# A fused decay-attention and two-MLP kernel: the seventh unit's gate moved behind the first MLP block, with the decays, loads and warming products around it reordered

## The reference

```python
f = 1.0 / (1.0 + np.exp(-f_logit))
for t in range(S):
    state = f[:, :, t, :, None] * state + np.einsum('bhd,bhe->bhde', k[:, :, t], v[:, :, t])
    y[:, :, t] = np.einsum('bhd,bhde->bhe', q[:, :, t], state)
...
x = y.transpose(0, 2, 1, 3).reshape(3072, 384)
x = (sigmoid(x @ w_gate) * (x @ w_val)) @ w_out          # d_ff 1536
h = x @ w_in                                             # d_ff 2048
out = (h * sigmoid(1.702 * h)) @ w_out2
```

## Time and profile before

| | |
|---|---|
| median of 3 runs | 955.58 us (955.3 to 957.54) |
| profiled execution, time | 953.83 us |
| its span (first to last instruction) | 952.1 us |
| mean granted TensorE clock | 0.988 of full |
| busy: TensorE, its weight loads | 930.8 us (98%), 778.2 us (82%) |
| busy: VectorE, ScalarE, GpSimd | 457.1 us (48%), 375.9 us (39%), 110.5 us (12%) |
| DMA | 52.36 MB, mean 55 GB/s |

### The profile page before, as it was taken

How to read it: one execution, slowest core, us unless ns; L and a number is a source line. 1 busy time by engine, 2 the same in 40 slices (tenths; PEclk the granted TensorE clock), 3 DMA queues, 4 the chain that set the end, 5 groups by cost and what they waited for, 6 DMA issues and landing times.

```text
span 952.1 us, 18119 instructions
## 1 busy us (share of the span) xinstructions
PE 930.8 (98%) x7179; PEld 778.2 (82%) x7179; DVE 457.1 (48%) x885; ACT 375.9 (39%) x917; POOL 110.5 (12%) x125
## 2 busy tenths in 40 slices
PE   7899989999999999999999999999999999999997
PEld 5799978888888888888888888888888888888885
DVE  7787655547545555654333234343443443443433
ACT  4665544444444444444324333333232233232232
POOL 3221211102111111210004420000000000000000
PEclk7899999999999999999999999999999999999999
DMA  5751322211212221120223320020010200100001
GB/s 146 224 167 55 86 66 60 64 48 29 85 45 59 75 57 50 26 76 26 63 67 100 99 83 1 1 67 0 24 44 1 67 1 0 67 1 1 34 0 36
DMA packets 44008, 52.36 MB, mean 55 GB/s; under 512 B 8464, under 2 KB 33808, under 8 KB 43920
## 3 DMA queue, kind: packets, MB, share of 16 engines
q1 hardware_dynamic: 41552, 43.58, 15.8%
q10 hardware_dynamic: 2368, 7.57, 2.6%
HBM read 36.96 MB, written 9.44 MB: 49 GB/s over the span
## 4 chain that ended last, share of the span: by engine, by line
PE 93%; DVE 2%; SPq 2%; ACT 1%; issue 1%; DMA 1%; POOL 0%; DVEq 0%; ACTq 0%; POOLq 0%
PE up_ps L1089 17%; PE up_ps L1091 17%; PE up_ps L1090 17%; PE out_ps L1089 13%; PE out_ps L1090 12%; PE out_ps L1091 12%; PE att_ps L1037 2%; PE att_ps L1059 1%; PE att_ps L1049 1%; PE turn_ps L1016 1%; PE att_ps L1082 1%; PE up_ps L1005 1%; SPq L410 1%; DMA f_raw<-f_t 1%; DVE after_prod L798 0%
## 5 line engine op out<-in xcount | busy, mean ns | idle before, releaser
L1089 PE MATMUL up_ps<-x_hi,w_hi 128*128 128x512 f32 (+1 forms) x792 | 294.8, 372 | 5.6 <-ACT act_f L704 4.9
L1091 PE MATMUL up_ps<-x_hi,w_lo 128*128 128x512 f32 (+1 forms) x792 | 294.4, 372 | 0.0
L1090 PE MATMUL up_ps<-x_lo,w_hi 128*128 128x512 f32 (+1 forms) x792 | 294.2, 371 | 0.0
L1089 PE MATMUL out_ps<-act_hi,w_hi 128*128 128x512 f32 (+1 forms) x540 | 207.9, 385 | 0.8 <-DVE act_lo L933 0.8
L1090 PE MATMUL out_ps<-act_lo,w_hi 128*128 128x512 f32 (+1 forms) x540 | 202.8, 375 | 0.0
L1091 PE MATMUL out_ps<-act_hi,w_lo 128*128 128x512 f32 (+1 forms) x540 | 202.4, 375 | 0.0
L710 ACT CAST act_hi<-act_f 128x512 fp32r<-128x512 f32 (+1 forms) x180 | 106.6, 592 | 233.8 <-DVE act_f L919 161.4
L1089 PEld LDWEIGHTS up_ps<-x_hi,w_hi 128*128 128x128 f32 x792 | 150.4, 190 | 31.7 <-issue 3.9
L1091 PEld LDWEIGHTS up_ps<-x_hi,w_lo 128*128 128x128 f32 x792 | 150.4, 190 | 25.4
L1090 PEld LDWEIGHTS up_ps<-x_lo,w_hi 128*128 128x128 f32 x792 | 150.5, 190 | 25.3
L933 DVE TENSOR_TENSOR act_lo<-act_f,act_hi 128x512 fp32r<-128x512 f32 (+1 forms) x180 | 118.2, 657 | 77.9 <-ACT act_hi L710 77.9
(11 more groups left out here) (78 smaller groups left out, 569.2 us busy)
## 6 DMA issues: line engine op xcount, KB each, us to landing
stage<-w SPq DMA_DIRECT2D x16, 384.0 KB, 3.2
stage<-w ACTq DMA_DIRECT2D x9, 576.0 KB, 4.7
k_raw<-k_t SPq DMA_DIRECT2D x96, 48.0 KB, 2.0
q_raw<-q_t SPq DMA_DIRECT2D x96, 48.0 KB, 1.9
v_raw<-v_n SPq DMA_DIRECT2D x48, 96.0 KB, 2.2
x_raw<-x_dram SPq DMA_DIRECT2D x6, 768.0 KB, 4.8
out_t<-final SPq DMA_DIRECT2D x18, 256.0 KB, 2.4
f_raw<-f_t SPq DMA_DIRECT2D x88, 48.0 KB, 1.9
```

Source lines behind the costliest of these rows:

```text
L1089: pe.matmul(dst, w_hi[:, at:at + P], m_hi, start=first, stop=False)
L1090: pe.matmul(dst, w_hi[:, at:at + P], m_lo, start=False, stop=False)
L1091: return pe.matmul(dst, w_lo[:, at:at + P], m_hi, start=False, stop=last)
```

## The change

In group 0 the gate of unit 6 (`forget(6)`) is no longer made ahead of block 0's sigmoid but in block 0 behind act_hi and prepare_q, and the later ones of the group follow, seven instead of six. The decays of group 0 are prepared in blocks 1, 3, 5, 7, 9, 11 (units 6 to 11) instead of 0, 1, 3, 5, 7, 9. `take_end` moves from the block that turns a unit to the block that prepares it, behind prepare_q and forget. SP issues load_kq ahead of load_v and move_y where the unit after the turned one was prepared in an earlier block (`early`), and load_v ahead of move_y always. In the first order of ScalarE load_w1(2) moves to its two fellows, forget(4) behind y's first moves, w1_first_part(1) ahead of x_first_part(0), forget(5) behind it. TensorE's first warming products are three instead of five, and two and three small ones follow visits 0 and 1. What is computed stays the same.

```diff
--- before.py
+++ after.py
@@ -71,14 +71,15 @@
     ahead_of = VISITS[VISIT_AT[0, 1]][0]
     for g in range(NG1 - 1):
         if g == 0:
-            forgets = {j: n + 2 for n, j in enumerate((0, 1, 2, 4, 6, 8))}
-            prepares = {j: n + 1 for n, j in enumerate((0, 1, 3, 5, 7, 9))}
+            forgets = {j: n + 1 for n, j in enumerate((0, 1, 2, 4, 6, 8, 10))}
+            prepares = {j: n + 1 for n, j in enumerate((1, 3, 5, 7, 9, 11))}
         else:
             forgets = {j: n + 3 for n, j in enumerate((0, 1, 3, 4, 5, 7, 8, 11))}
             prepares = {j: n + 2 for n, j in enumerate((0, 2, 3, 4, 6, 7, 10, 11))}
         FORGET_AT.update({(g, j): ahead_of + n for j, n in forgets.items()})
         PREPARE_AT.update({(g, j): ahead_of + n for j, n in prepares.items()})
         ahead_of += 5 if g == 0 else 8
+    PREPARE_BLOCK = {n: g * J1 + j for (g, j), n in PREPARE_AT.items()}
     SPLIT_AT1 = 10
     SPLIT_AT2 = 4
     AHEAD = 3
@@ -445,9 +446,11 @@
                 move_y(3, slice(1, None))
                 load_kq(5)
                 load_f(6)
+                load_v(4)
+                load_v(5)
                 load_f(7)
-                for n in range(4, 8):
-                    load_v(n)
+                load_v(6)
+                load_v(7)
                 load_kq(6)
 
                 for q in range(BLOCKS1):
@@ -456,12 +459,16 @@
                         store(b.g - 1)
                     if (b.g, b.j) in VISIT_AT:
                         turned, _, made = VISITS[VISIT_AT[b.g, b.j]]
+
+                        early = turned is not None and PREPARE_BLOCK.get(turned + 1, -1) < q
                         if turned is not None:
                             load_f(turned + 4)
+                        if early:
+                            load_kq(turned + 3)
                         if made is not None:
+                            load_v(made + 4)
                             move_y(made)
-                            load_v(made + 4)
-                        if turned is not None:
+                        if turned is not None and not early:
                             load_kq(turned + 3)
                     if b.g == NG1 - 2 and b.j == J1 - 1:
                         for t in range(STAGED):
@@ -673,11 +680,11 @@
                 prepare_q(1)
                 load_w1(0)
                 load_w1(1)
+                load_w1(2)
                 take_end(3)
                 take_k(3)
                 prepare_q(2)
                 take_y(0)
-                forget(4)
                 prepare_q(3)
                 take_y(1)
                 w1_first_part(0)
@@ -685,14 +692,14 @@
                 first_move_y(2, slice(0, 1))
                 take_y(3)
                 first_move_y(3, slice(0, 1))
-                load_w1(2)
+                forget(4)
+                w1_first_part(1)
+                x_first_part(0)
+                take_end(4)
                 forget(5)
-                x_first_part(0)
-                w1_first_part(1)
                 load_w1(3)
                 w1_first_part(2)
                 load_w1(4)
-                forget(6)
 
                 for q, b in enumerate(BLOCK):
                     if b.first_mlp:
@@ -713,13 +720,16 @@
                         turned, _, made = VISITS[VISIT_AT[b.g, b.j]]
                     if turned is not None:
                         take_k(turned)
-                        take_end(turned)
                     if made is not None and copied_first(out_visit[made]):
                         take_y(made)
                     if turned is not None:
                         prepare_q(turned)
                     if b.first_mlp and (b.g, b.j) in FORGET_AT:
                         forget(FORGET_AT[b.g, b.j])
+                    if b.q == 0:
+                        take_end(5)
+                    if b.first_mlp and PREPARE_AT.get((b.g, b.j), UNITS) < UNITS:
+                        take_end(PREPARE_AT[b.g, b.j])
                     if made is not None and not copied_first(out_visit[made]):
                         take_y(made)
                     if b.first_mlp and b.g == 0:
@@ -1001,7 +1011,7 @@
                         pe.matmul(up_ps[:, 0, 0:P], ident[:, :], ident[:, :], start=True, stop=True)
 
                 pe.wait_ge(warm_set, 1)
-                for _ in range(5):
+                for _ in range(3):
                     pe.matmul(up_ps[:, 0, 0:384], x_raw[:, 0, 0:P], x_raw[:, 0, 0:384], start=True, stop=True)
                 pe.wait_ge(consts_set, CONSTS)
 
@@ -1112,7 +1122,7 @@
 
                 for v in range(BEFORE_MLP):
                     visit(v)
-                    keep_warm({4: 2, 6: 8}.get(v, 0))
+                    keep_warm({0: 2, 1: 3, 4: 2, 6: 8}.get(v, 0))
 
                 for b in BLOCK:
                     q = b.q
```

## The result

The changed kernel takes 948.51 us (median of 9 runs, 947.42 to 950.62), the kernel before 954.87 us (9 runs; the ratio leaves out one slow run of 1038.23 us). The ratio is 0.9945, with a 95% interval of 0.9927 to 0.9963: 3.5 to 7 us faster, 6.4 by the medians. The profiled execution took 947.42 us, with a span of 945.7 us where before it was 952.1, 6.4 us less.

What follows compares the result with a forecast made beforehand. TensorE is busy from 140 us on, so its stalls and low clock ahead of that decide. 1.1 us lost up to group 1, then 3.1 + 3.7 gained: 5.7 us off 955.58 makes 949.9, range 944.8 to 956.5.

Steps and rivals of the forecast that it cites:

- The start: Head: fewer warming products and forget(4) later bring visit 5 forward by 1.5 us, bounds -0.2 and 2.8.
- The doubt about the clock: Head: shorter warming may delay the higher clock, at worst to 14 us, leaving -0.2 at visit 5; chance 0.14.
- Block 0: First block of group 0: starts near 24.8, 1.4 us earlier, its sigmoid no longer waiting for unit 6's gate.
- y's last copy (22.59, now 21.1): Head, ScalarE: the last copy of y ahead of block 0 comes at 21.1 instead of 22.59.
- x_hi is bound by the last moves landing: Block 0, ScalarE: x_hi waits for y's last moves, landing some 2.2 us after issue.
- q_dec at visit 9: Group 0: q_dec comes 5.9 us after mul(1), stalling TensorE 2.3 us; a clock fall costs 1.0 (0 to 2.2).
- The loop: Group 0, visits 9 to 12: late q_dec sets a pace of 9.45 us a visit instead of 8.45.
- The rival that it is no loop: Group 0: q_dec is in time or costs only visit 9; 3.5 us more stay, 946.4 us; chance 0.12.
- The copies: Group 1: earlier copies of the decays' ends remove waits for y_t, 3.1 us together (0 to 3.7).
- SP's queue: End of group 1: k and q ahead of y's move let the last move land earlier; 3.7 us, bounds 0 and 3.7.
- (d): Kernel before, at 136.29: block (2,0) waited 2.00 us, traced back to SP's last move of y landing late.
- The sum: Whole kernel: 1.1 us lost up to group 1, then 3.1 + 3.7 gained, 5.7 us in all.

Runs made afterwards that it cites:

- order back: Changed kernel with SP's order of before (move_y, load_v, load_kq) put back: 950.72 us, ratio 0.9968.
- five warming products: Changed kernel with five large warming products again and none behind visits 0 and 1: 948.46 us, ratio 0.9940.
- the head alone: Changed kernel with the copies of the decays' ends and SP's order both put back: 955.39 us, ratio 1.0011.
- earlier decays: Changed kernel with the decays of units 7 to 11 prepared in blocks 2, 3, 5, 7, 9 instead of 3, 5, 7, 9, 11: 944.85 us, ratio 0.9903.
- two parts: Kernel before with only the moved copies of the decays' ends and SP's new order from group 1 on: 947.01 us, ratio 0.9919.
- piece 2 late: Changed kernel with load_w1(2) issued behind ScalarE's first move of y, as before the change: 949.39 us, ratio 0.9952.

## Why the prediction was right, and where it was off

**The forecast** was 949.9 us, the measured median 948.51. Of these 1.4 us half is the start of the reckoning: it took 955.58 us for the kernel before, where nine runs gave 954.87. By the profiled spans 5.7 us were expected and 6.4 found. Step by step:

**The start** was right: 1.5 us expected at visit 5, 1.56 found, visit 0 at 5.82 for 5.8. The doubt about the clock was right in its mechanism and in its place: the clock is at half (0.50) from 8.7 to 12, and the visits pay for it, but it was back at 12 and not at 14.

**Block 0** was wrong: 24.8 expected, 26.64 found, and the block ran at half clock (0.50 from 26 to 31), so that block 1 started at 31.94 and not near 28. The step that failed is "y's last copy (22.59, now 21.1)". It took that copy to come 1.5 us earlier, with TensorE's visit; but the copy needs the slot of unit 0's y, whose moves leave late, and came at 22.63. Behind it the reckoning held: from VectorE's first scan of unit 4 to block 0 are 2.54 us, where 22.2 to 24.8 was forecast. "x_hi is bound by the last moves landing" was no bound: ScalarE began x_hi at 25.08 without a wait. Moving load_w1(2) ahead was booked as a pure gain; it gave its 0.9 us at the gate of unit 4 and cost 1.6 at the copy, 0.7 net. The other 1.30 us of the copy's wait stay without it.

**q_dec at visit 9** was right as a duration and wrong as a stall: from mul(1) at 34.92 to these products are 5.73 us (5.9 expected), but with TensorE itself late the stall was 0.99 us, not 2.3. In the four traces whose mean clock from 24 to 31 us was 0.84 or more and that kept the split first (order back, five warming products, the head alone, earlier decays) it was 2.32 or 2.33, as forecast. The clock did not fall there in the changed kernel's trace; in six of the other eleven kernels with this late gate it did, at 1.5 us where 1.0 (0 to 2.2) was taken. Why it stayed up in this one isn't shown.

**The loop** of visits 9 to 12 was right: 9.45 us a turn expected, 9.55 found, with 0.88 us of waiting each time. Group 0 ended 1.7 us behind, where 1.1 were forecast. The rival that it is no loop falls, and with the earlier decays the loop is gone.

**The copies** were right: 3.1 us expected, 3.2 found (3.7 of waits to 0.5), and 3.7 come back when they are put back.

**SP's queue** was right in the traces compared: the 2.00 us of (d) and 1.6 us of half clock are gone, 3.7 expected. Put back, it cost 2.2 us by the medians, and TensorE stood 2.16 us; with the copies back as well it stood 2.34. In both traces the clock stayed at 1.00 behind it, and only in the trace of the kernel before did it fall. So the clock's half of the price may or may not be paid, and that it was here is in part the luck of one trace.

**The sum** came out in part by luck. In the head 1.5 us were not won (2.7 expected at visit 9, 1.2 found: block 0 late and at half clock), and in their place 1.0 us that was foreseen did not come (the clock at visit 9); so group 0 missed its forecast by only 0.6 us. Group 1 carries the number, and its parts were right each: 6.8 us expected, 7.0 found. A further 1.1 us of the 6.4 lie behind it, and nothing in the forecast stands for them.

**Two of its signs.** "Block 1 starting near 28" did not come. One of the signs of being wrong did: ScalarE still waits for x_raw near 130, 0.83 us at 131.62 instead of 3.35. TensorE doesn't wait for it, so it costs nothing here, but it shows how little room SP's queue has.

## What to carry to other kernels

When a producer is moved nearer to its consumer, count the whole chain from the engine that frees it to the last of its products: k_dec was in time and q_dec, behind one more queue entry, was not, and that made a loop of 9.55 us out of 8.45. A load asked for earlier isn't free while small transfers on the critical path share the DMA engines; look for what waits for those to leave, also through a reused buffer. Where an issue is moved on a queue, book both ends: what it holds up where it goes, and what it lets through where it stood. Take a change of several parts apart before keeping it: here two parts gave 7.6 us and the others together nothing or less, until one table of block numbers, put right, made them worth some 2 us.

## What the runs showed of the hardware

The PEclk column read 1.00 from the first product on, in the kernel before and after, while the warming records ran 0.64 us apart for 384 columns, 0.21 for 128; sixteen records of 128 columns that began at a granted 0.50 took 0.18 each. That is the pace of 1.2 GHz. So the column seems to lack its first entry here, and the distance between records tells the level.

Which level the head's visits run at changes from run to run with nearly the same instructions: from 8 to 14 us the mean granted clock was 0.72 in the changed kernel, 1.00 with piece 3 of w1 early as well, and 0.60 with other block numbers for decays far behind. Much of it is absorbed in the head: with piece 2 late it was 0.72, with earlier decays added 1.00, visit 5 came at 17.79 and 19.03, and block 0 at 25.93 and 25.90.

GpSimd's multiply of 128x256 (two inputs in SBUF) took 0.68 us alone and 1.66 us beside VectorE's split of 128x1152, and the split 1.85 instead of 1.35 beside k_dec. By the Trainium skill (SBUF — State Buffer, section SBUF: two separate sides) a VectorE instruction with two SBUF inputs and a GpSimd instruction that reads SBUF share a port pair, which the one that starts first holds for its whole instruction while the other blocks. The trace agrees within 0.15 us: q_dec starts with 1.12 us of the split left and takes 0.98 longer, and the split starts with 0.63 us of k_dec left and takes 0.50 longer.
